# Scoring seven attention items in the first 18 steps and keeping their scores in device memory until their slots are free

## The reference

```python
batch, n_heads, seq, head_dim = 4, 8, 576, 64      # d_model 512, d_ff 2048, 2304 tokens, all float32
scores = scale * np.matmul(q, k.transpose(0, 1, 3, 2))
kth = np.partition(scores, -32, axis=-1)[..., -32:-31]
scores = np.where(scores >= kth, scores, -1e9)
scores = scores - np.max(scores, axis=-1, keepdims=True)
attn = np.exp(scores)
attn = attn / (np.sum(attn, axis=-1, keepdims=True) + 1e-9)
x = (attn @ v), heads side by side                  # 2304 x 512
h = x @ w_in;  x = np.maximum(0.01 * h, h) @ w_out  # first layer pair
h = x @ w_in2; g = h if h >= 1, 0 if h <= -1, else (h + 1)**2 / 4
return g @ w_out2                                   # second layer pair
```

## Time and profile before

| | us |
|---|---|
| median of 3 runs | 1164.52 (1164.34 to 1165.52) |
| the profiled execution | 1163.93 |
| its span (first to last instruction) | 1162.1 |
| busy: TensorE matmuls | 1092.6 (94%) |
| busy: VectorE | 877.2 (75%) |
| busy: ScalarE | 791.6 (68%) |
| busy: GpSimd | 464.8 (40%) |

### The profile page before, as it was taken

How to read it: one execution, slowest core, us unless ns; L and a number is a source line. 1 busy time by engine, 2 the same in 40 slices (tenths; PEclk the granted TensorE clock), 3 DMA queues, 4 the chain that set the end, 5 groups by cost and what they waited for, 6 DMA issues and landing times.

```text
span 1162.1 us, 21227 instructions
## 1 busy us (share of the span) xinstructions
PE 1092.6 (94%) x7568; PEld 1002.3 (86%) x7568; DVE 877.2 (75%) x1921; ACT 791.6 (68%) x1827; POOL 464.8 (40%) x493
## 2 busy tenths in 40 slices
PE   5457998899999999999999999999999999999998
PEld 3336887799988998899999879989998999999998
DVE  7999999889889998999979989888993005300234
ACT  7887999787788877887869868778885224322332
POOL 5654468552264432643225434225532234222322
PEclk9679999999999999999999999999999999999999
DMA  7988988697657788788667667565555677787764
GB/s 247 351 337 298 366 307 311 217 377 252 234 201 237 246 307 289 274 291 293 237 232 245 220 218 247 203 211 192 169 195 210 213 257 253 254 285 251 256 246 139
DMA packets 90680, 295.52 MB, mean 254 GB/s; under 512 B 10064, under 2 KB 13776, under 8 KB 90576
## 3 DMA queue, kind: packets, MB, share of 16 engines
q1 hardware_dynamic: 86544, 289.45, 71.2%
q10 hardware_dynamic: 4032, 4.72, 1.1%
HBM read 255.85 MB, written 38.27 MB: 253 GB/s over the span
## 4 chain that ended last, share of the span: by engine, by line
PE 69%; DVE 18%; ACT 5%; issue 3%; POOL 3%; DMA 1%; SPq 0%; POOLq 0%; ACTq 0%; DVEq 0%
PE ps_f L928 19%; PE ps_f L936 18%; PE ps_f L929 18%; DVE top L1211 8%; DVE work L1215 7%; PE ps_av L887 6%; PE ps_s L848 3%; PE ps_t L864 2%; DVE part_r L1238 2%; PE ps_t L870 2%; DMA raw<-wd 1%; PE ps_t L848 1%; POOL gate L741 1%; ACT probs L1056 1%; ACT probs L1048 1%
## 5 line engine op out<-in xcount | busy, mean ns | idle before, releaser
L1211 DVE MAX8 top<-work 128x8 f32<-128x576 f32 x432 | 310.2, 743 | 0.2
L928 PE MATMUL ps_f<-xy,w_ring 128*128 128x384 f32 (+2 forms) x896 | 289.3, 323 | 5.7 <-ACT gate L1115 2.0
L928 PE MATMUL ps_f<-gate,w_ring 128*128 128x384 f32 (+2 forms) x896 | 285.2, 318 | 0.0
L936 PE MATMUL ps_f<-gate,w_ring 128*128 128x384 f32 (+2 forms) x896 | 280.9, 314 | 4.1 <-POOL gate L741 4.0
L936 PE MATMUL ps_f<-xy,w_ring 128*128 128x384 f32 (+2 forms) x896 | 281.1, 314 | 1.6 <-POOL xy L751 1.1
L929 PE MATMUL ps_f<-xy,w_ring 128*128 128x384 f32 (+2 forms) x896 | 280.3, 313 | 0.0
L929 PE MATMUL ps_f<-gate,w_ring 128*128 128x384 f32 (+2 forms) x896 | 279.8, 312 | 0.0
L1215 DVE MATCH_REPLACE8 work<-top,work 128x576 f32<-128x576 f32 x288 | 213.3, 740 | 0.0
L741 POOL TENSOR_TENSOR gate<-part_r,gate 128x384 fp32r<-128x384 f32 (+2 forms) x112 | 101.3, 905 | 244.0 <-ACT gate L1115 243.9
L928 PEld LDWEIGHTS ps_f<-xy,w_ring 128*128 128x128 f32 x896 | 169.7, 189 | 19.9 <-issue 10.1
L928 PEld LDWEIGHTS ps_f<-gate,w_ring 128*128 128x128 f32 x896 | 169.2, 189 | 6.5 <-issue 6.2
(11 more groups left out here) (85 smaller groups left out, 1842.0 us busy)
## 6 DMA issues: line engine op xcount, KB each, us to landing
w_ring<-w_split SPq DMA_DIRECT2D x408, 512.0 KB, 4.2
w_split<-w_ring SPq DMA_DIRECT2D x40, 512.0 KB, 6.3
raw<-wd SPq DMA_DIRECT2D x64, 256.0 KB, 5.8
w_split<-xy SPq DMA_DIRECT2D x24, 512.0 KB, 5.0
v_sb<-vd SPq DMA_DIRECT2D x32, 320.0 KB, 5.7
kq<-kqd SPq DMA_DIRECT2D x16, 480.0 KB, 4.9
kq<-kqd SPq DMA_DIRECT2D x15, 416.0 KB, 3.6
out_t<-y_acc ACTq DMA_DIRECT2D x12, 192.0 KB, 4.3
```

The source lines that it names most:

```text
L928: pe.matmul(out, w[:, 0, m], high, start=first, stop=False)
L936: mm = pe.matmul(out, w[:, 0, m], low, start=False, stop=end)
L1211: op = dve.max(top[:, t % TOP_SLOTS, 8 * r:8 * r + 8], source(t, r))
```

## The change

A table gives seven items a step of their own: item 14 in step 8, 15 in 9, 16 in 11, 17 in 12, 18 in 13, 19 in 16 and 13 in 18. Their scores don't go to a slot of `scores`. ScalarE copies them into one of three stages, which are the buffers `part_r`, `part_o` and `y_acc` that only the layers use; SyncE stores them from there in `s_spilled` in device memory one step later, and loads them into their slot of `scores` in the step after the item seven before has been used (steps 19, 21, 23, 25, 26, 28 and 30). VectorE waits for that load in place of ScalarE's copy. All counting of scorings goes by the place in the new order (`PLACE`), and so do the loads of q and k: the groups are loaded in the order 0, 1, 2, 3, 6, 4, 7, 5, 8, and groups 8, 9 and 10 in steps 15, 17 and 19. In a step, the extra scoring stands last on TensorE, and the extra copy behind the exponential on ScalarE, ahead of the weight roundings. The first hidden unit waits until the stores from the stages are done.

```diff
+SPILLED_AT = {13: 18, 14: 8, 15: 9, 16: 11, 17: 12, 18: 13, 19: 16}
+SPILLED = list(SPILLED_AT)
+STAGES = 3
 def score_step(it):
+    if it.n in SPILLED_AT:
+        return SPILLED_AT[it.n]
...
+ORDER = sorted(ITEMS, key=lambda it: (score_step(it), it.n in SPILLED_AT))
+PLACE = {it.n: k for k, it in enumerate(ORDER)}
+REFILL_AT = {ITEMS[n - S_SLOTS].last + EXP_LAG + 1: n for n in SPILLED}
...
+            def store_spilled(it):
+                a = SPILL_ORDER.index(it.n)
+                sp.wait_ge(scores_copied, 2 * PLACE[it.n] + 2)
+                sp.dma_start(spilled(it, s_dram[a, :, :, :]),
+                             spilled(it, stages[a % STAGES])).then_inc(spill_stored[a % STAGES], 16)
+
+            def load_spilled(it):
+                a = SPILL_ORDER.index(it.n)
+                sp.wait_ge(spill_stored[a % STAGES], 16 * (a // STAGES + 1))
+                sp.wait_ge(kept, ITEMS[it.n - S_SLOTS].last + 1)
+                sp.dma_start(spilled(it, scores[:, it.n % S_SLOTS, :, :]),
+                             spilled(it, s_dram[a, :, :, :])).then_inc(spill_loaded[it.n % S_SLOTS], 16)
...
                     if s in OUT_AT:
                         transpose(OUT_AT[s])
+                    for it in SPILL_OF[s]:
+                        score(it)
...
             def copy_scores(it):
+                k = PLACE[it.n]
                 dst = scores[:, it.n % S_SLOTS, :, :]
+                if it.n in SPILLED_AT:
+                    a = SPILL_ORDER.index(it.n)
+                    dst = stages[a % STAGES]
+                    need(act, spill_stored[a % STAGES], 16 * (a // STAGES))
...
                     if t is not None:
                         exponential(t)
+                    for it in SPILL_OF[s]:
+                        copy_scores(it)
                     for a in direct_pieces(s):
                         high_direct(a)
...
+                    elif t == it.first and it.n in SPILLED_AT:
+                        earlier = [n for n in SPILLED if n <= it.n and n % S_SLOTS == it.n % S_SLOTS]
+                        dve.wait_ge(spill_loaded[it.n % S_SLOTS], 16 * len(earlier))
```

More of the change, by code:

```diff
@@ L270, in kq_loads, with kq_slot @@
 def kq_loads(gp):
-    return gp // KQ_SLOTS + (gp % KQ_SLOTS > 0)
+    return KQ_PLACE[gp] // KQ_SLOTS + (KQ_PLACE[gp] % KQ_SLOTS > 0)
+def kq_slot(gp):
+    return KQ_PLACE[gp] % KQ_SLOTS
 def kq_parts(gp):
@@ L497, in build @@
     w_dram = nc.dram_tensor("w_split", [PIECES, P, 2, PIECE], F32, kind="Internal").ap()
+    s_dram = nc.dram_tensor("s_spilled", [len(SPILLED), P, 2, S], F32, kind="Internal").ap()
     with ExitStack() as ctx:
@@ L552, in build @@
         out_stored = sem("out_stored")
+        spill_stored = [sem("spill_stored%d" % a) for a in range(STAGES)]
+        spill_loaded = [sem("spill_loaded%d" % a) for a in range(S_SLOTS)]
         zeroed = sem("zeroed")
@@ L587, in score_halves, with spilled @@
         def score_halves(it):
-            return [ps_s, ps_f[:, 0:2, :] if it.n < SCORED_EARLY else ps_late]
+            return [ps_s, ps_f[:, 0:2, :] if PLACE[it.n] < SCORED_EARLY else ps_late]
+        def spilled(it, where):
+            return where[:, 0:it.tiles, :]
         def x_parts(gp):
@@ L626, in load_kq @@
             def load_kq(gp):
[L627 to L631, removed]
-                first, end = kq_span(gp)
-                sp.dma_start(kq[:, gp % KQ_SLOTS, first:end], kqd[gp, :, first:end]).then_inc(kq_loaded[gp % KQ_SLOTS], 16)
+                if KQ_PLACE[gp] >= KQ_SLOTS:
+                    old = KQ_ORDER[KQ_PLACE[gp] - KQ_SLOTS]
+                    if old >= FIRST_ROUNDED:
+                        sp.wait_ge(kq_low_done, 2 * (old - FIRST_ROUNDED + 1))
+                    else:
+                        sp.wait_ge(scores_done, 2 * LAST_PLACE[old] + 2)
+                first, end = kq_span(gp)
+                sp.dma_start(kq[:, kq_slot(gp), first:end], kqd[gp, :, first:end]).then_inc(kq_loaded[kq_slot(gp)], 16)
+            def store_spilled(it):
[9 more added lines that the diff above has]
+                             spilled(it, s_dram[a, :, :, :])).then_inc(spill_loaded[it.n % S_SLOTS], 16)
             def load_v(gp):
@@ L680, in _ @@
             for s in range(len(PLAN)):
-                if s in KQ_LOAD_AT:
-                    load_kq(KQ_LOAD_AT[s])
+                for gp in KQ_LOAD_AT[s]:
+                    load_kq(gp)
+                if s:
+                    for it in SPILL_OF[s - 1]:
+                        store_spilled(it)
+                if s in REFILL_AT:
+                    load_spilled(ITEMS[REFILL_AT[s]])
                 if s in V_LOAD_AT:
@@ L757, in low_kq @@
                 slot = kq_split[:, gp % KQ_HALVES, :, first:end]
-                pool.tensor_tensor(slot[:, 1, :], kq[:, gp % KQ_SLOTS, first:end], slot[:, 0, :].bitcast(F32),
+                pool.tensor_tensor(slot[:, 1, :], kq[:, kq_slot(gp), first:end], slot[:, 0, :].bitcast(F32),
                                    ALU.subtract).then_inc(kq_low_done, 1)
@@ L822, in score @@
             def score(it):
-                if it.n == 0:
+                k = PLACE[it.n]
+                if k == 0:
                     pe.wait_ge(kq_first, 32)
@@ L1107, in read_bank @@
                     act.wait_ge(gate_low_done[old.layer], old.in_layer + 1)
+                if u.h == 0:
+                    for a in range(min(STAGES, len(SPILLED))):
+                        act.wait_ge(spill_stored[a], 16 * len(range(a, len(SPILLED), STAGES)))
                 slot = u.h % G_SLOTS
```

49 lines of the change are left out of this document (29 added, 20 removed).

## The result

| | before | after |
|---|---|---|
| median of 4 runs each, side by side on one chip | 1165.02 us (1164.34 to 1165.63) | 1178.7 us (1178.26 to 1180.48) |
| ratio, 95% interval | 1 | 1.012 [1.0104, 1.0136] |
| profiled execution: span | 1162.1 us | 1176.5 us |

The change makes the kernel 1.2% slower, 13.7 us of medians. The sign, the mechanism and the range of the prediction hold; its point, 1175.3 us, is 3.4 us too low, and two terms behind it were mis-sized.

The account below looks back on a forecast made before the run. VectorE was taken to bound up to 160 us, then ScalarE, with TensorE setting the end. A 13.5 us delay less 2.7 returned gives +10.8 on 1163.9, 1174.7, plus 0.6 to the median: 1175.3 us; range 1164 to 1180 us.

Parts of the forecast that it names:

- What bounds the kernel: VectorE's top-k up to 160 us, then ScalarE; TensorE's work between 91 and 184 us is not on the path.
- The delay of the first stage, step by step: Steps 8 to 18: ScalarE waits for spilled scores and copies them, delaying VectorE by 10.1 to 15.3 us.
- its scoring "at the low clock" at 7.33 us: Scoring on TensorE used for sizing: first copy 1.4 us after its start, second half an estimated 1 us later.
- The choice of 13.5 between 10.1 and 15.3: VectorE enters the layers 13.5 us late, taken between the high-clock sum of 10.1 and the step-by-step sum of 15.3.
- the 10.1 us that I had worked out by it: First stage: added matmuls raise TensorE's clock themselves, so the delay would be 10.1 us.
- What comes back, "1.1 + 1.7 = 2.7 us": From 160 to about 205 us ScalarE leads and no longer copies items 18 and 19: 2.7 us back.
- TensorE's 8.2 us turn into waits: Steps 24 to 34: the seven scorings removed from TensorE, 8.2 us, become waits and bring nothing back.
- DMA at nothing beyond the lateness: First stage: 4.5 MB of added transfers, 12 us, are covered by ScalarE's lateness; without it they would be a delay.
- The first (TensorE is the bound in the layers): TensorE is the bound from 104 us on, so its 8.2 us count: +5.3, 1169.8 us; chance 0.15.
- The second (the stage absorbs the copies, and the kernel gets faster): First stage absorbs copies, delaying VectorE only 1.5 us, and 8.2 come back: -6.7, 1157.8 us; chance 0.12.
- The third (DMA): First stage: stores ahead of raw weights make these land later, a third of 12 us more: +14.8, 1179.3 us; chance 0.08.

Follow-up runs that it names:

- experiment 3: Kernel before with the scoring matmuls of items 13 to 19 cut from 288 to 16 columns, in their old places: 1164.06 us, ratio 1.000.
- experiment 7: Kernel before without any scoring matmul for items 13 to 19: 1164.1 us, ratio 0.9995.
- experiment 1: Changed kernel with the extra item scored first on TensorE in steps 9, 11, 13, 16 and 18: 1169.97 us, ratio 1.005.
- Experiment 4: Kernel before with scoring matmuls and ScalarE's copies of items 13 to 19 both cut to 16 columns: 1164.61 us, ratio 1.0005.
- experiment 8: Kernel before with four weight roundings of the first stage moved from ScalarE to GpSimd, nothing spilled: 1162.83 us, ratio 0.9991.
- Experiment 2: Changed kernel with transfers of the spilled scores cut from 576 to 64 columns, every wait kept: 1178.4 us, ratio 1.0126.
- experiment 5: Changed kernel with scoring first as in experiment 1, and copies and transfers of the spilled items cut to 16 columns: 1166.8 us, ratio 1.002.

## Why the prediction was right, and where its sizes were off

**What bounds the kernel** was right. The chain is on VectorE from 107 to 177 us as it was from 74 to 160, and TensorE's seven scorings in the layers are off the path (experiments 3 and 7).

**The delay of the first stage, step by step.** Ends of the steps on ScalarE (starts of the rows shown above against the earlier trace rows) and closes on VectorE (against the earlier trace rows), as a lag:

| | predicted | measured |
|---|---|---|
| before step 8 | 0 | 0.5 (23.83 against 23.28) |
| step 8 | +1.9 | +2.5 (41.97 against 39.49) |
| step 9 | +4.6 | +6.1 (50.68 against 44.57) |
| step 12 | +7.0 | +7.9 (67.66 against 59.73) |
| step 13 | +10.9 | +11.9 (75.56 against 63.71) |
| close at 73.78 us | +10.9 | +11.4 (85.13) |
| close at 83.61 us, behind step 16 | 2.2 more | 2.3 more (97.23) |
| last close, behind step 18 | 2.2 more, 15.3 | 2.1 more, 15.7 (106.30) |

The walk along the order was right within 0.1 us in what steps 8, 13, 16 and 18 add. Step 9 added 0.9 us more than was put down for it, and steps 11 and 12 added 0.6 less. In step 9 I had taken 3.6 us for the value products, "mostly at the low clock", from a stretch whose mean granted clock was 0.63 (40.80 to 44.41 us); in the changed kernel it is 0.50 there (43.30 to 47.76), and they took 4.46 us. The waits of ScalarE for items 15 and 18 were put at 2 to 3 us and were 3.67 and 2.85. The half microsecond ahead of step 8 was in no term. It arises by 23.83 us, before any moved item is scored, and experiment 1 has the same loads up to there and none of it, so it stays unexplained.

One row is misread in the prediction: for its scoring "at the low clock" at 7.33 us the profile gives a granted clock of 1.00 (7.30 to 9.70 us). The sizes taken from it hold all the same: that matmul's 0.84 us is what the same instruction takes at 40.48 us in experiment 1, where the granted clock is 0.50.

**The choice of 13.5 between 10.1 and 15.3** is the first step that failed: "more low than high, so I take 13.5". 15.7 us were measured, which is the sum with the low clock (15.3). Granted clocks as means over a window did not say which instructions get which level. From 34 to 64 us the mean rose from 0.61 to 0.67, from 64 to 91 it stayed at 0.75, and still the two groups of value products on the path took 3.68 and 3.27 us, each behind an idle gap of 3 us. That the gap is the reason is likely from experiment 1 but not proven: its third group took 3.05 us with no gap ahead. The rule of the Trainium skill ("TensorE: Matmul & The Clock Gate", "Part 1: The HAM clock gate"), that activity releases the clock, agrees with experiment 1, where the scoring came just ahead of the products (2.52 and 1.95 us), but not with the 10.1 us that I had worked out by it for the change: there the added matmuls stand behind the products, and did nothing for them.

**What comes back, "1.1 + 1.7 = 2.7 us"** is the second step that failed. It rested on ScalarE leading the chain from 160 to 205 us. Experiment 4 takes these copies away and gains nothing (1.0005, and at most 0.8 us by its interval): the rows on ScalarE in the chain were places at which the chain passed through, not work whose length set the end. The 1.4 us that the profiled execution did get back (15.7 less the 14.3 of lag at 240 us of before's time) come with the clock of one group of value products. They aren't work that the change saves; whether the change's delay brings that clock is open (experiment 8). Without this, 15.7 + 1163.9 and the 0.6 to the median would have given 1180.2 us, 1.5 above what was measured, which is again the size of that difference.

**TensorE's 8.2 us turn into waits**: right in that they bring nothing, experiments 3 and 7. Its idle time itself grew by 5.9 us, in windows that are 1 us longer. **DMA at nothing beyond the lateness**: right. The prediction added that without the lateness the transfers would be a delay themselves. Experiment 2 doesn't test that, as it is as late as the change. Experiment 1 speaks against it: with full transfers and 6.4 us of lag ScalarE waits 2.0 us for raw weights, and going on to small transfers and short copies (experiment 5) takes off 3.0 us of lag, no more than the 3.5 us that it takes off in the order of the change.

**The rivals.** The first (TensorE is the bound in the layers) fell with experiment 7: its 8.2 us would have been 0.7%, and the interval ends at 0.9986. In the changed kernel TensorE does run ahead there, being 4.8 us less late than VectorE at 158 us of before's time, but by 173 us it waits and the lead is down to 0.8. The second (the stage absorbs the copies, and the kernel gets faster) needs both halves, and neither holds: with nearly all of ScalarE's waits gone the kernel is still slower by 0.5% (experiment 1), and the return is zero. The rule of the Trainium skill on which it drew ("Perfetto Trace Analysis", "Identifying the Most-Contended Engine"), to begin with the engine of highest occupancy, does not hold for this edit when it is read over the whole span: TensorE was busy for 94% of it, and 8.2 us less of its work at this place were worth nothing. Read within the stage it agrees, since VectorE is the fullest engine from 91 to 160 us (68.83 us against TensorE's 63.40). The third (DMA) fell with experiment 2 and ScalarE's shorter waits for raw weights.

**Left open.** The last 0.2% of the corner with scoring first and short copies. Its trace has 3.2 us of waits of ScalarE for items 14 and 17 in steps 8 and 12, which is about its lag of 3.4 us; no run takes these two waits away, so that they are the 0.2% is argued, not shown. Open too is whether the fast group at 216.66 us is an effect of the delay, and how the order's 8 us divide between the wait for the scores and the clock of the products.

## What to carry to other kernels

An engine's idle share says that work would fit, not that its consumer gets it in time: before work is moved into a half-empty stage, write down for each step what stands ahead of it in its queue, and what that waits for. Here, in the two steps that cost most, the scoring stood behind products that waited for the very engine which then waited for the scores, and the order as a whole cost 8 us, more than twice the copies. And ask first what the place that is relieved is worth: a variant that simply leaves the work out there costs one run, and would have shown that there was nothing to win.

## What the runs showed of the hardware that was not expected

The same group of 16 value products (128x256) takes 3.68 us in one order and 2.52 in another in step 9, and 3.27 and 1.95 in step 13, with only the place of the scorings changed; the slow ones are those where TensorE had been idle for some 3 us just ahead, the fast ones those where scorings filled that gap. It isn't the whole rule: the third group of experiment 1 took 3.05 us behind scorings. For the 128x320 groups it is 2.37 and 3.71 us, and 4.07 in experiment 7 for the group at 200.39 us. Of the unchanged kernel 21 runs beside experiments 1 to 4 spread from 1160.81 to 1166.6 us; steps of 1.3 to 1.7 us by such groups are of a size to make up a good part of this, which was seen only in the traces compared here. The Trainium skill ("TensorE: Matmul & The Clock Gate", "Part 1: The HAM clock gate") calls the time at which the clock rises variable from run to run. The 21 runs agree in so far as the mean granted clock of one and the same kernel lies between 0.977 and 0.987 in them. It goes with the time only in part: the two runs at 0.977 are the slowest (1166.31 and 1166.6 us), the three at 0.987 took 1162.55 to 1162.91, but the fastest, 1160.81 us, is one of eight at 0.984.

DMA shares of 0.99 at 383 GB/s from 104 to 175 us, 338 GB/s before, held VectorE up nowhere: of its 2.2 us of gaps there 1.99 are the close at 106.30 us, none of its waits is for a load of scores, and its lag is 15.7 us at 110 us and 15.8 at 173. A reload of 576 KB that takes 10.2 us to land was early enough.
